# The lead-in of a fused attention and experts kernel in another order: loads on two queues, spans from index fills, one trigonometric stay, and products between TensorE's sums

## Chip, cores and metric

The kernel runs on one core of a Trainium2 chip. The metric is the device time of one execution in microseconds; lower is better.

## What is computed

Attention with a complex decay over 4 x 8 heads, 768 positions, 48 columns, in float32:

```
mag = sqrt(a_re*a_re + a_im*a_im);  scale = min(mag, 0.999) / (mag + 1e-6)
for t in range(S):                       # a = (a_re + i a_im) * scale
    S_re, S_im = a * (S_re + i S_im) + k[t] outer v[t]   # the product is real, added to S_re
    y[t] = q[t] @ S_re
```

Its output becomes 3072 rows of 384. Every row is given to one of 8 experts of 384 rows each, in the order of the scores `x @ w_gate`, and passes `relu(x @ w1[e]) @ w2[e]`. Last, all rows pass `((x @ w_a) * (x @ w_b)) @ w_out`.

## The kernel before, in words

The program has two blocks, attention and experts. The change is in the first (function `attention`, from L185), and there almost wholly in what each engine does ahead of its loop.

**Tiles.** A tile `g` is 128 positions of all 8 heads of one batch: 24 tiles. The recurrence inside of a tile is written as products. Decays are kept as logarithms: `log_r` (L1226) is the log of the clipped magnitude, its sums over positions are products with triangular constants (`to_mid`, `mid_to_end`, `spans`; L864, L868, L876), and `exp` of these sums scales queries and keys. The phase is summed in the same way in turns (`sum_phase`, L880 to L892: a product with `tri_turns`, one with `tri_half`, one with `last_row`), reduced to half a turn (L1246, L1250), and its sine and cosine turn queries and keys (L531, L532). Keys and queries are transposed (`turn`, L856), copied (L625, L626), scaled by the spans (`scale`, L1149 and three times L1162), and multiplied block by block at four distances (`gram_near`, L915, `gram8`, `gram16`, `gram32`, L926, L937, L947). `mask` (L1193) keeps the causal half.

**Pairs.** What depends on `a` alone is made for a pair `m` of tiles, 768 columns wide: squares (L680, L686), their sum (L1199), log (L652), magnitude (L663), log of the magnitude plus a small number (L657), the denominator |re| + magnitude (L667, L1205), its inverse as exp(-ln) with one correction (L672, L674, L1210, L1212), the ratio (L1256), its arctangent (L711), and the angle (L1240), with `left` (L1232) for the negative half plane.

**Order.** There is no scheduler. Each engine has a list written out by hand: `start()`, then a loop of ten passes with two tiles each (`body` with a late, a middle and an early tile), then `finish()`. Engines hand over by semaphores counted per tile or pair; an engine works through its own list in order, so a wait holds all that stands behind it. ScalarE's table holds either log and exp or sine and arctangent; `to_trig` and `to_exp` (L730, L733) load the other. The first body of TensorE begins with the turn of tile 1; that of VectorE with the scaling of tile 1.

**The lead-in.** SP issues the loads: pair 0 of `a` (four parts of 192 KB), pair 1, then `wg` and `w_out`'s first tile, and after a wait for VectorE's zeroing (`zeroed`) q, k and v of tiles 0 and 1. TensorE waits for `wg` ahead of its first product (L845). GpSimd makes all constants first: `first_constants`, `sum_constants`, `other_constants` (L258 to L279). The last of these makes `spans`, 66 columns of ones cut by 16 selects, each waiting for the one before. TensorE's first span sums wait for all of them (L1011, `const_made` at 3).

ScalarE's `start()` (L735) squares both halves of pairs 0 and 1, and makes pair 1's log and magnitude ahead of tile 0's decays; VectorE's is at L1259, TensorE's at L1007, GpSimd's at L575. The lines in question are these, with their surroundings:

## Time and profile before

| what | us |
|---|---|
| median of 3 runs | 1132.54 |
| the three runs | 1132.19, 1132.54, 1135.49 |
| the profiled execution, its own time | 1136.5 |
| its span, first to last instruction | 1134.8 |
| busy TensorE, VectorE, ScalarE, GpSimd | 1063.5, 813.2, 505.9, 446.9 |
| attention's loop, from and to about | 51, 383 |

A profile shows one execution. The page sums it up by engine, by slices of the span, by the chain that ended last and by groups of instructions. The order of time lists instructions with start, duration, line and tiles, and in brackets how long the engine had been idle and what ended that. The table of stretches gives each engine's busy time in stretches of the span, and the granted clock of TensorE, 1.00 for 2.4 GHz and 0.50 for 1.2 GHz.

### The profile page before, as it was taken

The numbers are of one execution on the slowest core, as the hardware profiler recorded it, in microseconds if no ns is written. First come the engines' busy times: TensorE is split into PE (matmuls) and PEld (weight loads), VectorE is DVE, ScalarE is ACT, GpSimd is POOL, SyncE is SP. The second block draws the span as 40 slices with busy tenths as digits, with TensorE's granted clock in tenths as the row PEclk, the third lists the DMA queues.
The fourth block names the chain that finished last, engine by engine and source line by source line (L and its number), as shares of the span: only waits on it lengthen the run. The fifth ranks groups of instructions, "written<-read, shape, count | busy, mean of one in ns | idle before, by whom it ended". The sixth has DMA issues, their size and how long they took to land.

```text
span 1134.8 us, 36403 instructions
## 1 busy us (share of the span) xinstructions
PE 1063.5 (94%) x14126; PEld 978.1 (86%) x14126; DVE 813.2 (72%) x1808; ACT 505.9 (45%) x951; POOL 446.9 (39%) x473
## 2 busy tenths in 40 slices
PE   1899999999999927899999999999999999999997
PEld 1578888888888816899999999999999999999997
DVE  5779999999998887865865865865864864874221
ACT  6767777777776332224323323323323323313322
POOL 7556565555566326703403403403403502502501
PEclk9989999999999958999999999999999999999999
DMA  6233444444433153030030030030030030030000
GB/s 133 57 69 83 88 90 90 90 90 90 90 85 83 32 174 133 29 115 19 21 111 22 21 111 22 21 111 22 21 111 22 21 111 22 14 118 22 21 1 21
DMA packets 163640, 73.99 MB, mean 65 GB/s; under 512 B 140016, under 2 KB 158192, under 8 KB 163568
## 3 DMA queue, kind: packets, MB, share of 16 engines
q1 hardware_dynamic: 160496, 63.73, 21.4%
q0 software_dynamic: 3072, 9.44, 2.6%
q8 instruction: 28, 0.46, 0.2%
q14 instruction: 44, 0.36, 0.1%
HBM read 63.71 MB, written 9.44 MB: 64 GB/s over the span
## 4 chain that ended last, share of the span: by engine, by line
PE 58%; DVE 3%; issue 1%; DMA 1%; ACT 0%; POOL 0%; SPq 0%; DVEq 0%; ACTq 0%; POOLq 0%
PE tb L2196 26%; PE acc L1837 7%; PE acc L1839 7%; PE acc L1838 7%; PE tb L1837 2%; PE tb L1839 2%; PE tb L1838 2%; PE ps_r L1747 1%; DVE slot L152 1%; DVE thr L145 1%; DMA w1s<-in_moe_w 1%; PE tb L1820 0%; PE tb L2149 0%; PE tb L2153 0%; PE tb L2150 0%
## 5 line engine op out<-in xcount | busy, mean ns | idle before, releaser
L2018 ACT CAST ab_high<-ab 128x384 fp32r<-128x384 f32 x96 | 49.4, 514 | 224.5 <-DVE ab L2103 211.0
L2103 DVE TENSOR_TENSOR ab<-tb,a_sb 128x384 f32<-128x384 f32 x96 | 53.3, 556 | 100.4 <-PE tb L2196 95.1
L1886 POOL TENSOR_TENSOR w_low<-w1s,w_high 128x384 fp32r<-128x384 f32 x64 | 65.6, 1034 | 144.2 <-ACT w_high L1963 144.2
L1810 POOL DMA_INDIRECT xg<-x_rows,tok_next x24 | 25.7, 1070 | 221.8 <-issue 221.5
L2196 PE MATMUL tb<-x_high,wb_high 128*128 128x384 f32 x288 | 99.7, 346 | 0.0
L1837 PE MATMUL acc<-wo_high,ab_high 128*128 128x384 f32 x288 | 98.2, 341 | 0.3 <-DVE ab_low L2106 0.3
L2196 PE MATMUL tb<-x_high,wa_high 128*128 128x384 f32 x288 | 97.5, 338 | 0.0
L1839 PE MATMUL acc<-wo_high,ab_low 128*128 128x384 f32 x288 | 97.4, 338 | 0.0
L1838 PE MATMUL acc<-wo_low,ab_high 128*128 128x384 f32 x288 | 97.1, 337 | 0.0
L2106 DVE TENSOR_TENSOR ab_low<-ab,ab_high 128x384 fp32r<-128x384 f32 x96 | 53.6, 558 | 60.1 <-ACT ab_high L2018 60.1
L2196 PE MATMUL tb<-x_high,wb_low 128*128 128x384 f32 x288 | 96.6, 335 | 0.0
L2196 PE MATMUL tb<-x_high,wa_low 128*128 128x384 f32 x288 | 96.5, 335 | 0.0
L2014 ACT COPY a_sb<-tb 128x384 f32<-128x384 f32 x96 | 46.0, 479 | 112.8 <-PE tb L2196 112.8
L1162 DVE TENSOR_TENSOR x<-ps_t,span_dec 112x512 f32<-112x512 f32 x144 | 90.0, 679 | 0.0
L152 DVE TENSOR_TENSOR slot<-best,thr 128x768 bf16<-128x768 f32 (+1 forms) x80 | 88.2, 1121 | 0.9
L557 POOL TENSOR_TENSOR kxt<-rot,to_end 128x384 f32<-128x384 f32 x48 | 48.4, 1032 | 100.5 <-DVE log_r L1226 50.3
L1892 POOL TENSOR_TENSOR w_low<-w2s,w_high 128x384 fp32r<-128x384 f32 x64 | 72.5, 1133 | 37.7 <-ACT w_high L1974 37.4
L2034 DVE SCALAR_TENSOR_TENSOR hid_low<-tb,hid_high 128x384 fp32r<-128x384 f32 x64 | 35.4, 554 | 58.3 <-ACT hid_high L2000 57.5
L1837 PE MATMUL acc<-hid_high,w_high 128*128 128x384 f32 x192 | 66.9, 349 | 1.4 <-DVE hid_low L2034 1.4
L524 POOL TENSOR_TENSOR qk_dec<-qk,dec 128x384 f32<-128x384 f32 x48 | 57.4, 1196 | 23.3 <-ACT dec L632 22.9
L2196 PE MATMUL tb<-x_low,wa_high 128*128 128x384 f32 x288 | 65.6, 335 | 0.0
L2196 PE MATMUL tb<-x_low,wb_high 128*128 128x384 f32 x288 | 65.4, 334 | 0.0
(371 smaller groups left out, 3019.0 us busy)
## 6 DMA issues: line engine op xcount, KB each, us to landing
w1s<-in_moe_w SPq DMA_DIRECT2D x8, 1536.0 KB, 6.4
w2s<-in_moe_w SPq DMA_DIRECT2D x8, 1152.0 KB, 9.4
a_re_in<-in_a_re SPq DMA_DIRECT2D x30, 192.0 KB, 3.1
a_im_in<-in_a_im SPq DMA_DIRECT2D x30, 192.0 KB, 3.7
qk<-in_q SPq DMA_DIRECT2D x24, 192.0 KB, 2.7
qk<-in_k SPq DMA_DIRECT2D x24, 192.0 KB, 3.3
vv<-in_v SPq DMA_DIRECT2D x48, 96.0 KB, 2.9
x_rows<-ysb SPq DMA_DIRECT2D x24, 192.0 KB, 3.0
```

The costliest lines, as they stand in the source:

```text
L152: return v.tensor_tensor(t["slot"][:, cols, :], scores[:, cols].unsqueeze(2).broadcast_to([P, n, NTH]), t["thr"][:, min(i, 1), :].unsqueez ...
L524: nc.gpsimd.tensor_tensor(qk_dec[:, :, cs], qk[:, u, :, cs], dec[:, :, cs], ALU.mult).then_inc(s["qk_decayed"], 1)
L1162: nc.vector.tensor_tensor(view(xw[n][:, hs, :]), mixed, by, ALU.mult).then_inc(s[f"scaled{w}"], 1)
L1837: nc.tensor.matmul(out_ap, left[0], right[0], start=start, stop=False)
L1838: nc.tensor.matmul(out_ap, left[0], right[1], start=False, stop=False)
L1839: return nc.tensor.matmul(out_ap, left[1], right[0], start=False, stop=stop)
L1886: nc.gpsimd.tensor_tensor(w1p[1][:, f % NW1, :, :], w1_tile(f), w1p[0][:, f % NW1, :, :].bitcast(F32), ALU.subtract).then_inc(s["w1_low"], 1)
L1892: nc.gpsimd.tensor_tensor(w2p[1][:, f % 2, :], w2s[:, f, :], w2p[0][:, f % 2, :].bitcast(F32), ALU.subtract).then_inc(s["w2_low"], 1)
L2018: nc.scalar.copy(abp[0][:, f % 2, :], ab[:, f % 2, :]).then_inc(s["ab_high"], 1)
L2103: nc.vector.tensor_tensor(ab[:, f % 2, :], tb[(2 * f + 1) % 4][:, 0:CAP], a_sb[:, f % 2, :], ALU.mult).then_inc(s["ab_made"], 1)
L2106: nc.vector.tensor_tensor(abp[1][:, f % 2, :], ab[:, f % 2, :], abp[0][:, f % 2, :].bitcast(F32), ALU.subtract).then_inc(s["ab_low"], 1)
L2196: mm = nc.tensor.matmul(tb[(2 * f + m) % 4][:, 0:CAP], w[:, k, :], x[:, k, :], start=(n == 0), stop=(n == len(terms) - 1))
```

## The change

- **Loads.** SP issues only the real parts of pair 0, then q and k of tile 0, then pair 1; ScalarE's queue issues the imaginary parts of pair 0 as its first act. q and k of tile 1 and the v loads come after `w_out`'s tile. The zeroing of `vv` is split in two halves and moved behind the first square sum and the second imaginary square on VectorE; each v load waits for its half.
- **Spans.** The 16 selects go. 16 index fills write two sides into a buffer that isn't in use yet, without waits between them; VectorE takes the minimum and compares with 0. TensorE waits for that (`spans_ready`) in place of all constants.
- **Squares.** VectorE makes the imaginary squares of pairs 0 and 1, ScalarE the rest.
- **ScalarE's list.** Inversion of pair 0 is split around the square of pair 1. Tile 0's decays and span decays come ahead of pair 1's size, log and magnitude. The two arctangents stand side by side; `log_magnitude_eps(1)` goes behind the reload of the log table; the size of pair 2 goes out of the stay with the sine table.
- **TensorE.** Six products of 384 columns whose result nobody reads, between the span sums and the first phase sum, and one between the two phase sums; some steps of tile 0 change places.
- **VectorE.** Another order of `start()`: the square sum of pair 2 behind the second angle, `log_twice_capped(2, 0)` ahead of `scale(0, 0, 1)`, `log_decay(1, 1)` ahead of `denominator(2)`, `left_side(2, 0)` and `square_sum(3)` last.
- **GpSimd.** Its wait for the ratio of pair 2 ahead of tile 1's keys goes.

The core of the diff:

```diff
@@ SP
-                load_a(sp, 0, 0, 0, 0)
+                load_part(sp, a_re, re_in, 0, 0, 0)
+                load_qk(sp, 0, 0, 0)
                 load_a(sp, 1, 0, 2, 1)
                 sp.dma_start(wg[:], w_gate.rearrange("(n p) e -> p n e", p=P)).then_inc(gate_loaded, 16)
                 load_wo(sp, 0)
-                sp.wait_ge(zeroed, 1)
+                load_qk(sp, 0, 1, 1)
                 for u in range(2):
-                    load_qk(sp, 0, u, u)
+                    sp.wait_ge(zeroed, u + 2)
                     load_v(sp, 0, u, u)
@@ GpSimd
                 def start():
                     sum_constants(pool)
+                    span_sides(pool, sides)
                     other_constants(pool)
...
                     queries_and_keys(1, 1, 0)
-                    pool.wait_ge(s["ratio_made"], after("ratio_made", 2))
                     keys_to_end(1, 1)
+    def span_sides(pool, sides):
+        def side(view, pattern, base, cm):
+            nc.gpsimd.iota(view, pattern=pattern, base=base, channel_multiplier=cm, **kw).then_inc(sides_made, 1)
@@ ScalarE
+                load_part(act, a_im, im_in, 0, 0, 0)
                 nc.scalar.preload_act_table_set("natural_log_exp_and_others")
...
                     square_re(0, 0)
-                    square_im(0, 0)
                     absolute(0, 0)
                     log_magnitude(0)
                     magnitude(0)
                     log_magnitude_eps(0)
+                    act.wait_ge(s["den_made"], after("den_made", 0))
+                    nc.scalar.activation(den_inv[:], den[:], ACT.Ln).then_inc(s["den_logged"], 1)
                     square_re(1, 1)
-                    square_im(1, 1)
-                    inverse(0)
+                    act.wait_ge(s["den_logged"], after("den_logged", 0))
+                    nc.scalar.activation(den_inv[:], den_inv[:], ACT.Exp, scale=-1.0).then_inc(s["log_den_inv"], 1)
+                    decays(0, 0)
+                    span_decays(0, 0, 0)
+                    span_decays(0, 0, 1)
+                    absolute(1, 1)
                     log_magnitude(1)
                     magnitude(1)
-                    decays(0, 0)
-                    log_magnitude_eps(1)
-                    absolute(1, 1)
-                    span_decays(0, 0, 0)
-                    span_decays(0, 0, 1)
                     inverse(1)
                     to_trig()
                     arctan(0)
+                    arctan(1)
                     square_re(2, 0)
+                    half_sines(0, first_sines)
                     square_im(2, 0)
-                    absolute(2, 0)
-                    arctan(1)
-                    half_sines(0, first_sines)
                     half_sines(1, s["sines_made"])
                     act.sem_inc(s["cos_abs"], 1)
                     copy_turned(0, 0)
                     to_exp()
-                    decays(1, 1)
+                    log_magnitude_eps(1)
+                    decay_to_mid(1)
                     copy_turned(0, 1)
+                    decay_of_end(1)
+                    absolute(2, 0)
                     span_decays(1, 1, 0)
                     log_magnitude(2)
+                    span_decays(1, 1, 1)
                     magnitude(2)
-                    span_decays(1, 1, 1)
@@ TensorE
+                def keep_running(products):
+                    for _ in range(products):
+                        nc.tensor.matmul(ps_u[:, 0, 0:HD], to_mid[:], log_r[:, 0, :], start=True, stop=True)
...
-                    pe.wait_ge(const_made, 3)
+                    pe.wait_ge(spans_ready, 2)
                     sum_spans(0, 0, 0)
                     pe.wait_ge(s["ends_made"], after("ends_made", 0))
                     sum_spans(0, 0, 1)
+                    keep_running(FIRST_RUN)
                     sum_phase(0, 0, None, ps_y)
+                    keep_running(1)
                     sum_phase(0, 1, None, ps_y)
                     sum_mids(1, 1, 0)
                     sum_ends(1, 1)
                     turn(0, 0)
+                    gram_near(0, 0)
                     sum_phase(1, 0, None, ps_y)
-                    gram_near(0, 0)
+                    turn(0, 1)
                     gram8(0, 0)
                     gram16(0, 0)
-                    turn(0, 1)
                     gram32(0, 0)
@@ VectorE
+                def make_spans():
+                    dve.wait_ge(sides_made, 4 * len(LEVELS) + 4)
+                    nc.vector.tensor_tensor(spans[:], sides[0], sides[1], ALU.min).then_inc(spans_ready, 1)
+                    dve.wait_ge(spans_ready, 1)
+                    nc.vector.tensor_scalar(spans[:], spans[:], 0.0, None, ALU.is_ge).then_inc(spans_ready, 1)
                 def start():
+                    square_im(0, 0)
                     square_sum(0)
+                    nc.vector.memset(vv[:, 0, :, :, :], 0.0).then_inc(zeroed, 1)
+                    log_twice_capped(0, 0)
                     denominator(0)
-                    log_twice_capped(0, 0)
                     log_decay(0, 0)
+                    left_side(0, 0)
+                    square_im(1, 1)
+                    nc.vector.memset(vv[:, 1, :, :, :], 0.0).then_inc(zeroed, 1)
+                    make_spans()
+                    invert(0)
                     square_sum(1)
-                    invert(0)
                     ratio(0, 0)
-                    left_side(0, 0)
+                    denominator(1)
                     log_twice_capped(1, 1)
-                    denominator(1)
                     invert(1)
                     angle(0)
                     ratio(1, 1)
-                    square_sum(2)
                     reduce_phase(0, 0, ps_y)
                     reduce_phase(0, 1, ps_y)
                     left_side(1, 1)
                     angle(1)
+                    square_sum(2)
                     scale(0, 0, 0)
                     reduce_phase(1, 0, ps_y)
+                    log_twice_capped(2, 0)
                     scale(0, 0, 1)
                     reduce_phase(1, 1, ps_y)
+                    log_decay(1, 1)
                     denominator(2)
-                    log_decay(1, 1)
-                    log_twice_capped(2, 0)
                     dve.wait_ge(const_made, 3)
                     mask(0)
-                    square_sum(3)
-                    left_side(2, 0)
                     invert(2)
                     ratio(2, 0)
+                    left_side(2, 0)
+                    square_sum(3)
```

`FIRST_RUN` is 6.

## Rows read from the trace of the kernel before

**Rows 1.** The page, part 4: the chain that ended last, shares by engine.

```profile
PE 58%; DVE 3%; issue 1%; DMA 1%; ACT 0%; POOL 0%; SPq 0%; DVEq 0%; ACTq 0%; POOLq 0%
```

**Rows 2.** Table of stretches: us, busy us per engine (instructions), granted clock, DMA share, GB/s.

```profile
75.00:103.50 28.50, 28.19 (x798) 23.15 (x797) 26.09 (x38) 21.62 (x38) 18.98 (x17) 1.00 0.40 88
```

**Rows 3.** Order of time, VectorE: start us, duration us, line, operation; log_r.

```profile
49.49 0.95 DVE L1226 SCALAR_TENSOR_TENSOR log_r<-log_twice,log_mag_eps 128x768 f32<-128x768 f32 x1
...
87.86 0.95 DVE L1226 SCALAR_TENSOR_TENSOR log_r<-log_twice,log_mag_eps 128x768 f32<-128x768 f32 x1
...
354.98 0.95 DVE L1226 SCALAR_TENSOR_TENSOR log_r<-log_twice,log_mag_eps 128x768 f32<-128x768 f32 x1
```

**Rows 4.** Table of stretches of 2 us in the first pass.

```profile
58.00:60.00 2.00, 1.74 (x49) 1.64 (x41) 1.88 (x4) 1.63 (x4) 0.84 (x2) 0.50 1.14 223
...
68.00:70.00 2.00, 1.99 (x94) 1.86 (x91) 1.88 (x4) 0.39 (x1) 0.00 (x0) 1.00 0.72 179
```

**Rows 5.** Order of time, TensorE, in the first and the second pass.

```profile
53.20 0.81 PE L868 MATMUL ps_r<-log_r,mid_to_end 128*128 128x384 f32 x2
...
54.69 0.69 PE L915 MATMUL ps_s<-qd,kd 112*64 112x64 f32 x16 [0.69 <-ACT kd L626]
...
57.37 0.74 PE L926 MATMUL ps_s<-x 112*8 112x8 f32 x64 [1.98 <-DVE x L1162]
...
58.64 1.95 PE L856 MATMUL ps_t<-ident,rot 128*112 128x128 f32 x8 [0.26 <-DVE x L1162]
...
66.44 1.18 PE L891 MATMUL ps_r<-phase,last_row 128*128 128x384 f32 x2
...
92.34 1.08 PE L856 MATMUL ps_t<-ident,rot 128*112 128x128 f32 x8
...
96.64 0.81 PE L891 MATMUL ps_r<-phase,last_row 128*128 128x384 f32 x2
```

**Rows 6.** The first load: order of time, and one row of the stretches.

```profile
2.09 1.95 SPq L432 DMA_DIRECT2D a_im_in<-in_a_im  x2
...
2.18 1.28 ACT L617 ACT_TABLE_LOAD   x1 [2.18 <-issue]
...
3.50:4.00 0.50, 0.00 (x0) 0.00 (x0) 0.47 (x3) 0.00 (x0) 0.43 (x2) 1.00 1.09 216
```

**Rows 7.** Order of time from the first square to the first span sums.

```profile
6.69 0.84 ACT L680 ACTIVATE mag<-a_re_in 128x768 f32<-128x768 f32 x1 [3.23 <-DMA a_im_in<-in_a_im]
...
8.93 9.71 POOL L222 TENSOR_SCALAR_AFFINE_SELECT spans<-spans 128x8 f32<-128x8 f32 x16
...
13.09 0.96 DVE L1226 SCALAR_TENSOR_TENSOR log_r<-log_twice,log_mag_eps 128x768 f32<-128x768 f32 x1
...
21.29 1.15 PE L876 MATMUL ps_e<-spans,log_r 128*64 128x66 f32 x16 [4.09 <-POOLq L279]
...
24.58 0.14 POOL L166 IOTA weight<- 128x8 f32 x1
```

**Rows 8.** Order of time, first angle, and one phase sum at either level.

```profile
25.37 1.28 ACT L730 ACT_TABLE_LOAD   x1
...
27.60 0.96 DVE L1240 SCALAR_TENSOR_TENSOR theta<-left,arc 128x768 f32<-128x768 bf16 x1 [0.26 <-ACT arc L711]
...
28.61 1.65 PE L889 MATMUL ps_y<-theta,tri_turns 128*128 128x384 f32 x2 [5.29 <-DVE theta L1240]
...
30.37 1.49 PE L891 MATMUL ps_y<-phase,last_row 128*128 128x384 f32 x2
...
45.73 0.91 PE L889 MATMUL ps_y<-theta,tri_turns 128*128 128x384 f32 x2
```

**Rows 9.** Order of time, tile 0 copied and scaled, tile 1 scaled.

```profile
38.98 0.56 ACT L625 COPY qd<-ps_t 112x512 f32<-112x512 f32 x1
...
44.69 0.69 DVE L1149 TENSOR_TENSOR qs<-ps_t,span_dec 112x512 f32<-112x512 f32 x1 [1.49 <-ACT qd L625]
...
56.03 0.68 DVE L1149 TENSOR_TENSOR qs<-ps_t,span_dec 112x512 f32<-112x512 f32 x1
```

More of the change, by code:

```diff
@@ L51 @@
 WARM_UP = 16
+FIRST_RUN = 6
 BETWEEN_TILES = (2, 2, 1)
@@ L299, in attention @@
         turns = sbi("turns", [P, HD])
+        sides = [turns[:, n * NSPAN:(n + 1) * NSPAN] for n in range(2)]
         cos_sin = sbi("cos_sin", [P, 2, 2, HD])
@@ L416, in load_v, with load_part @@
                     sp.dma_start(vv[ts, u, :, j, :], src[ts, :, :]).then_inc(v_loaded[u], 16)
+            def load_part(eng, x, dst, b, c, parity):
+                for i in range(2):
+                    to = dst[:, parity, i, :] if isinstance(parity, int) else \
+                        dst[:, bass.ds(parity, 1), i, :].rearrange("p o n -> p (o n)")
+                    eng.dma_start(to.rearrange("p (h d) -> p h d", h=H), chunk(x, b, c if i == 0 else c + 1)
+                                  ).then_inc(a_loaded, 16)
             def load_a(sp, m, b, c, parity):
@@ L428, in load_a @@
                 for x, dst in zip((a_re, a_im), a_in):
[L429 to L433 removed]
+                    load_part(sp, x, dst, b, c, parity)
             def store(sp, g, u):
```

47 lines of the change are left out of this document (26 added, 21 removed).

## The prediction, made before the changed kernel ran

> **What bounds the kernel now.** I read the page first, then the table of stretches, then the order of time of the lead-in. On the page the chain that ended last is 58% TensorE [rows 1]: the second half, the experts, is a TensorE stream that the change doesn't touch. The attention loop decides what a lead-in is worth. Its stretches are full on TensorE (28.19 of 28.50 us) with VectorE close behind (26.09) [rows 2], so each engine takes from the lead-in only a starting time, and one microsecond of later start is one microsecond of later end. The pace is in log_r, made once per pass: 49.49, 87.86, and nine passes later 354.98 [rows 3]. Later passes take (354.98 - 87.86) / 9 = 29.68 us, the first 38.37, so 8.7 us are lost in it. Where, is in the clock column: 0.50 at 58 to 60, 1.00 at 68 to 70 [rows 4]. Ahead of that fall TensorE has little to do: the sums of ends finish at 54.01, 0.69 us of products stand at 54.69, and the next begin at 57.37, 1.98 us of that wait for VectorE's scaled tile [rows 5]. The fall's price comes from the same work in two passes [rows 5]: from the turn at 58.64 to the end of the phase sums at 67.62 is 8.98 us, from 92.34 to 97.45 it is 5.11. So **the fall costs 3.9 us**. Note that the clock column shows 1.00 at 3.5 us as well [rows 6], ahead of TensorE's first product and of any record; a product of one shape takes 1.65 us at 28.61 and 0.91 at 45.73 [rows 8], so TensorE still stood at its lower level (1.2 GHz) at 28.61.
>
> **The change, step by step.** Times are from the start of the profiled span; "now" is the trace.
> 1. First load. Now SP issues all four parts, the last two from 2.09 on, and the first square starts at 6.69 [rows 6, 7]. At 3.5 to 4.0 us the DMA engines move 216 GB/s at a share of 1.09 [rows 6]: they are full, and 0.197 MB takes 0.9 us. Issuing from two queues can't speed up what the engines bound. ACT can't issue ahead of 2.18 [rows 6], and SP now sends q and k of tile 0 (0.39 MB) in between. Bounds: landing as now (6.65) if these stay behind, 8.5 if both go ahead (2 x 0.9 more). I take 8.0, as they alternate. The Trainium skill (DMA: Bandwidth & Descriptors, Queues, rings and completion order) says that each engine goes round the queues with work packet by packet; by that rule, as an estimate, the two loads on ACT's queue land near 7.8, and the sum would be 0.2 us better.
> 2. To the first log_r. Now the step from the square at 6.69 to log_r's end at 14.05 takes 7.36 [rows 7]. With the imaginary square on VectorE beside ScalarE's, and the capped log ahead of the denominator: three VectorE steps of 0.96 and three of ScalarE near 0.87, with their hand-overs 5.8 us: 13.8. TensorE can't start earlier, for wg is behind the second load on SP, which waits for the first: 1.35 later than now. TensorE starts at 14.2, as now to 0.1 us. Gain here: nothing. VectorE's two added squares (1.9 us) and the zeroing of vv (1.3 us, in two halves, moved from ahead of the load to behind it) lie in its waits for ScalarE; without these waits they would cost 3.2 us.
> 3. Spans. Now 16 selects hold GpSimd for 9.71 us and the span sums start at 21.29 [rows 7]. Sixteen index fills at 0.14 to 0.2 us each [rows 7] take 3.2 at most and are made by 12; the small minimum and compare on VectorE, not in the trace, are bounded by 0.1 and 0.5 each; I take 0.12, as the width is 66 against the 768 of a 0.96 us step. They are done by 16.2, hidden behind the decays, which end near 16.9. Span sums start at 16.9 and end by 19.0: **4.3 us earlier**.
> 4. But the second pair's size, log and magnitude are put behind these spans on ScalarE. Size 19.4, log 20.2, magnitude 21.1 to 21.9, denominator to 22.9, two inversions to 24.6, table load (1.28) to 25.9, arctangent, angle to 27.7; now it ends at 27.60 + 0.96 = 28.56 [rows 8]. **Of 4.3 us 0.85 are left.**
> 5. TensorE kept running: a phase sum is five passes of 384 columns and takes 3.25 us now, 28.61 to 31.86 [rows 8], so 0.65 a pass at the lower level. Six products of two passes take 7.8, from 19.0 to 26.8, ahead of the angle at 27.7: cover 0.9 us, and if it goes, what is over is a delay. Now TensorE is idle for 5.29 us ahead of 28.61 [rows 8] and both phase sums of tile 0's pair run at the lower level; with TensorE busy from 17 on I take the clock as full when the first one starts. Each then takes 0.91/1.65 of 3.25, 1.8 us: 2.9 us for two. Turning of tile 0's first half ends at 35.35, where it is 38.9 now (its copy starts at 38.98 [rows 9]): 3.5 us earlier.
> 6. What is late next: VectorE's second scaling of tile 0. Now it starts at 44.69 [rows 9]. The change puts log_twice of pair 2 ahead of it. On ScalarE stand, from 35.4: two copies, table load, the log moved out of the first stay, two decays (to 39.3), two copies to 40.8, the end decay, a size, a span decay, then pair 2's log, ending at 43.1. log_twice ends at 44.1, and the scaling starts there: **0.6 us ahead of now**; the other 2.9 us are VectorE's new wait.
> 7. The tail of the lead-in to the scaling of tile 1 is now 44.69 to 56.03, 11.3 us of full VectorE [rows 9]. After: 2.5 scaling, 1.1 reduction, log_r, denominator, mask to 50.0; then it waits for two ScalarE inversions (1.8 us behind a denominator that comes second instead of first) until 51.2, three steps to 54.1, side and square sum: 55.4. Again 0.6 ahead. The same walk made for the kernel before gives 55.1 where the trace has 56.0, so it is up to 0.9 short; if that lag is whole in the new order too, this is a loss of 0.3. I take the middle, **-0.2 us**, with -1.5 (first load as now) and +1.6 (latest load, whole lag) as ends.
> 8. At nothing: the wait that GpSimd loses (tile 1's keys are wanted only by the state's products late in the first pass), and the v loads, each now behind its half of the zeroing (the later at 15.7) and behind it the loads of pair 2: these wait for pair 0's ratio at 19.6 as well and land near 25.3, where the first square of pair 2 stands at 29.5. That is a cover of 4 us; if it goes, ScalarE waits with the sines behind it.
>
> Against the profiled execution's own 1136.5 the sum is 1136.3, the fall left in. The median of the runs shown is 4.0 us lower than that execution, and of three runs two lie at 1132.2 and 1132.5 and one at 1135.5. That is the size of the fall, so perhaps the fall isn't in each execution; the runs have no trace to show it. The median goes to 1132.54 - 0.2 = 1132.3.
>
> **Rivals.**
> Slower: the fall comes in nearly every execution. In the new order TensorE is through with the sums of ends by about 52, two microseconds sooner, since log_r is made ahead of the denominator; the next big work is still bound to VectorE's scaling at 55.4, so it begins near 56.8. The poor stretch is 4.8 us with 0.7 of products in it, where it is 3.4 now [rows 5]. If the runs at 1132 had no fall, it adds 3.9: 1136.2. It decides where that stretch is longer than now. For it: the arithmetic of steps 6 and 7. Against: two of three runs of before may have passed such a stretch without a fall. The Trainium skill (TensorE: Matmul & The Clock Gate, HAM oscillation) says that waits between bursts bring the lower level back, each time anew; by that rule too the time is that of this rival, and rows 4 and 5 agree with it at one place.
> Faster: the fall goes, because with the clock full early TensorE's work lies elsewhere, and the median of before had it (the profile's 4.0 us then being the profiler's). 1132.3 - 3.9 = 1128.4. For it: the fall stands behind one stretch only, and a scaling of tile 1 that comes two microseconds sooner than step 7 has it would close that stretch. Against: step 7 finds no such gain.
> The products don't do what they are for: the clock is still at the lower level in both phase sums. Then the 2.9 us of step 5 come back: 1135.2. Against: TensorE is busy from 17 on, where now it is idle until 28.6.
>
> **How the numbers follow.** Forecast 0.46 (own range 1130.8 to 1134.1), slower rival 0.27, faster rival 0.22, idle products 0.05. A measurement of this kernel tells 0.3% (3.4 us) from no change: under 1129.1 is faster, over 1135.9 slower. The slower rival lies on that line, 0.17 of it beyond; with the 0.05 slower is 0.22 at most. Faster is the rival and 0.03 of the forecast's tail: 0.25. The rest, 0.53, is the same. The range takes in both rivals' times: 1128.0 to 1136.8.
>
> **What would show it.** In the new profile: first square at 7.8 to 8.2 (step 1); span sums by 17.5 (3); first angle ending near 27.7 (4); phase sums under 1.8 us from the first on (5); VectorE idle some 3 us until log_twice near 43, second scaling at 44 (6); scaling of tile 1 at 55.4 to 56.4 (7); and the clock column between 50 and 70, with the first pass's 38.4 us, says which rival holds. Wrong would be a first pass that starts before 54 or after 57.5, or a later pass that isn't 29.7 us long: then the lead-in does something to the loop that I haven't seen.

## The result, and the profile after

| | before | after |
|---|---|---|
| median (8 executions each, in turn on one chip) | 1133.24 us | 1137.80 us |
| range | 1132.19 to 1135.49 | 1135.23 to 1140.25 |
| ratio after / before | | 1.0038, 95% interval 1.0024 to 1.0052 |
| profiled execution, own time / span | 1136.5 / 1134.8 | 1139.83 / 1138.1 |
| mean granted clock of that execution | 0.979 | 0.975 |

The change makes the kernel slower by 0.38%, some 4.3 us. I had forecast 1132.3, range 1128.0 to 1136.8; the result lies outside. Of the 5.5 us between forecast and result 0.7 are the base, since the kernel before took 1133.24 here. Measured once more on another chip (the run after_again below) the ratio is 1.0034 [1.0021, 1.0046].

The page of after, parts 1, 2 and 4. Every engine has nearly the work it had, and the chain's shares are those of [rows 1].

```profile
PE 1070.7 (94%) x14140; PEld 983.0 (86%) x14140; DVE 816.3 (72%) x1813; ACT 505.6 (44%) x949; POOL 442.2 (39%) x472
...
PEclk9889999999999967999999999999999999999999
...
PE 58%; DVE 3%; issue 2%; DMA 1%; POOL 0%; ACT 0%; DVEq 0%; POOLq 0%; ACTq 0%; SPq 0%
```

First load to first span sums, order of time. These rows answer to [rows 6, 7].

```profile
2.18 1.08 ACTq L431 DMA_DIRECT2D a_im_in<-in_a_im  x2
...
7.67 0.84 ACT L700 ACTIVATE mag<-a_re_in 128x768 f32<-128x768 f32 x1 [3.10 <-DMA a_im_in<-in_a_im]
...
9.29 1.94 POOL L265 IOTA turns<- 128x8 f32 x16 [0.17 <-POOL end_bias L258]
...
12.49 0.96 DVE L1253 SCALAR_TENSOR_TENSOR log_r<-log_twice,log_mag_eps 128x768 f32<-128x768 f32 x1
...
13.71 1.62 PE L886 MATMUL ps_e<-log_r,to_mid 128*128 128x384 f32 x2 [13.71 <-POOLq L287]
15.56 0.16 DVE L1294 TENSOR_TENSOR spans<-turns 128x66 f32<-128x66 f32 x1
15.76 0.20 DVE L1296 TENSOR_SCALAR spans<-spans 128x66 f32<-128x66 f32 x1
...
16.54 1.15 PE L898 MATMUL ps_e<-spans,log_r 128*64 128x66 f32 x16
```

Pair 1's steps, the products and the first phase sum; they answer to [rows 8]. The two VectorE steps of 1.64 and 1.75 us take 0.95 elsewhere; GpSimd's `qk_dec` runs beside them.

```profile
16.41 2.94 POOL L537 TENSOR_TENSOR qk_dec<-qk,dec 128x384 f32<-128x384 f32 x2 [2.85 <-ACT dec L650]
...
16.85 1.64 DVE L1239 SCALAR_TENSOR_TENSOR den_inv<-den,den_inv 128x768 f32<-128x768 f32 x1
...
18.41 1.75 DVE L1226 SCALAR_TENSOR_TENSOR mag<-mag,im 128x768 f32<-128x768 f32 x1
18.50 4.75 PE L1031 MATMUL ps_u<-log_r,to_mid 128*128 128x384 f32 x12
...
26.98 0.96 DVE L1267 SCALAR_TENSOR_TENSOR theta<-left,arc 128x768 f32<-128x768 bf16 x1 [0.26 <-ACT arc L731]
...
27.99 1.65 PE L911 MATMUL ps_y<-theta,tri_turns 128*128 128x384 f32 x2 [4.75 <-DVE theta L1267]
```

Now the place where the time goes. It answers to [rows 9] and [rows 3].

```profile
36.48 1.65 DVE L1267 SCALAR_TENSOR_TENSOR theta<-left,arc 128x768 f32<-128x768 bf16 x1
...
37.27 1.72 POOL L545 TENSOR_TENSOR rot<-qk_dec,cos_sin 128x384 f32<-128x384 f32 x1
38.05 1.76 DVE L1226 SCALAR_TENSOR_TENSOR mag<-mag,im 128x768 f32<-128x768 f32 x1
38.94 2.69 POOL L570 TENSOR_TENSOR kxt<-rot,to_end 128x384 f32<-128x384 f32 x2
39.73 0.68 DVE L1176 TENSOR_TENSOR qs<-ps_t,span_dec 112x512 f32<-112x512 f32 x1
...
42.25 1.09 PE L878 MATMUL ps_t<-ident,rot 128*112 128x128 f32 x8 [1.52 <-DVE x L1189]
...
43.38 0.59 ACT L639 COPY qd<-ps_t 112x512 f32<-112x512 f32 x1 [2.03 <-PE ps_t L878]
...
45.82 0.86 ACT L672 ACTIVATE log_mag<-mag 128x768 f32<-128x768 f32 x1
...
46.71 1.06 DVE L1245 SCALAR_TENSOR_TENSOR log_twice<-log_mag 128x768 f32<-128x768 f32 x1 [3.46 <-ACT log_mag L672]
47.69 0.68 DVE L1176 TENSOR_TENSOR qs<-ps_t,span_dec 112x512 f32<-112x512 f32 x1
...
51.14 0.95 DVE L1253 SCALAR_TENSOR_TENSOR log_r<-log_twice,log_mag_eps 128x768 f32<-128x768 f32 x1
...
58.94 0.68 DVE L1176 TENSOR_TENSOR qs<-ps_t,span_dec 112x512 f32<-112x512 f32 x1
...
89.44 0.95 DVE L1253 SCALAR_TENSOR_TENSOR log_r<-log_twice,log_mag_eps 128x768 f32<-128x768 f32 x1
...
356.55 0.95 DVE L1253 SCALAR_TENSOR_TENSOR log_r<-log_twice,log_mag_eps 128x768 f32<-128x768 f32 x1
```

Read it backwards. The second scaling of tile 0 starts at 47.69, where it was 44.69. It stands behind `log_twice`, which waits 3.46 us for ScalarE's log of pair 2. That log is late because ScalarE's two copies before it wait for TensorE's second turn. The turn waits for VectorE's first scaling, and that one stands behind an angle and a square sum of 1.65 and 1.76 us, beside GpSimd's `rot` and `kxt`. In the kernel before, the same copies and the same log stood at nearly the same time:

```profile
44.07 0.58 ACT L625 COPY qd<-ps_t 112x512 f32<-112x512 f32 x1 [1.40 <-PE ps_t L856]
...
45.65 0.83 ACT L652 ACTIVATE log_mag<-mag 128x768 f32<-128x768 f32 x1
```

There the scaling waited for the copies alone. What is new is that it waits for the log as well.

From the second scaling on the lag stays: tile 1 is scaled at 58.94 (56.03 before). At `log_r`, which now stands ahead of the denominator, the lag is smaller: 1.65 us at the first of the loop (51.14 against 49.49) and still 1.57 at the last (356.55 against 354.98). So the loop itself has its old pace, (356.55 - 89.44) / 9 = 29.68 us a pass.

The span has grown by 3.3 us, though, so 1.7 us more are lost **behind** the last `log_r`, in work the change doesn't touch. The tables of stretches, after and then before, show what is different there: the clock falls once more, where it didn't before.

```profile
394.00:396.00 2.00, 1.34 (x10) 1.37 (x11) 1.86 (x4) 0.00 (x0) 0.00 (x0) 0.81 0.02 6
396.00:398.00 2.00, 2.00 (x20) 1.83 (x21) 0.47 (x1) 0.00 (x0) 0.00 (x0) 0.50 0.03 8
```

```profile
392.00:394.00 2.00, 2.00 (x35) 1.91 (x34) 1.36 (x3) 0.00 (x0) 0.00 (x0) 1.00 0.00 0
```

It falls in the state's products, which wait 1.13 us for VectorE in both kernels: 16 of them take 2.76 us in after and 1.78 before.

```profile
394.66 2.76 PE L922 MATMUL ps_u<-vv,kxt 128*112 128x96 f32 x16 [1.13 <-DVE state L1211]
```

```profile
391.72 1.78 PE L900 MATMUL ps_u<-vv,kxt 128*112 128x96 f32 x16 [1.13 <-DVE state L1184]
```

### The profile page after: what moved, and what is told of

It reads as the page before. It is cut to its first block, busy times and chain, and to the rows that moved or that the text cites. A ratio compares the mean times of both kernels' runs of the same rounds, so it can differ in the third digit from the quotient of the medians.

```text
span 1138.1 us, 36431 instructions
## 1 busy us (share of the span) xinstructions
PE 1070.7 (94%) x14140; PEld 983.0 (86%) x14140; DVE 816.3 (72%) x1813; ACT 505.6 (44%) x949; POOL 442.2 (39%) x472
## 4 chain that ended last, share of the span: by engine, by line
PE 58%; DVE 3%; issue 2%; DMA 1%; POOL 0%; ACT 0%; DVEq 0%; POOLq 0%; ACTq 0%; SPq 0%
PE tb L2240 27%; PE acc L1881 7%; PE acc L1883 7%; PE acc L1882 7%; PE tb L1881 2%; PE tb L1883 2%; PE tb L1882 2%; PE ps_r L1791 1%; DVE slot L153 1%; DVE thr L146 0%; PE tb L1864 0%; PE tb L2193 0%; PE tb L2197 0%; PE tb L2194 0%; DMA w2s<-in_moe_w 0%
## 5 line engine op out<-in xcount | busy, mean ns | idle before, releaser
L2078 DVE SCALAR_TENSOR_TENSOR hid_low<-tb,hid_high 128x384 fp32r<-128x384 f32 x64 | 35.5, 555 | 58.4 <-ACT hid_high L2044 57.5
```

## The experiments

Four theories. **Order**: VectorE's two moves (the square sum of pair 2 ahead of the first scaling, `log_twice` ahead of the second) cost it. **Port**: VectorE's steps with two inputs in SBUF meet GpSimd. **Clock**: TensorE's poor stretches bring the lower level back, ahead of the loop and near 395. **Products**: the six products are too few, or harmful. Each kernel was timed in five rounds beside the kernel before on the same chip. An execution of the kernel before took 1129.7 to 1140.9 us in these jobs, with medians from 1134.2 to 1135.1, so ratios within 0.002 of each other aren't told apart. Ratio and median can differ by up to 0.0013, as in undo_three; the argument goes by the ratio. The last three columns come from one profiled execution each.

| run | ratio [95%] | median | 2nd scaling of tile 0 | tile 1 scaled | last log_r |
|---|---|---|---|---|---|
| (before, profiled execution) | 1 | | 44.69 | 56.03 | 354.98 |
| (after, first measurement) | 1.0038 [1.0024, 1.0052] | 1137.80 | 47.69 | 58.94 | 356.55 |
| after_again | 1.0034 [1.0021, 1.0046] | 1138.81 | 48.05 | 59.29 | 356.88 |
| twice_back | 1.0028 [1.0016, 1.0041] | 1137.35 | 44.23 | 57.50 | 357.00 |
| square_back | 1.0046 [1.0030, 1.0062] | 1140.45 | 47.28 | 58.78 | 358.17 |
| undo_two | 1.0015 [0.9996, 1.0034] | 1137.07 | 44.14 | 57.20 | 353.65 |
| undo_three | 1.0003 [0.9985, 1.0021] | 1136.64 | 43.43 | 57.16 | 355.97 |
| undo_four | 1.0010 [0.9992, 1.0028] | 1135.02 | 42.86 | 56.18 | 352.08 |
| wait_alone | 1.0013 [0.9995, 1.0030] | 1136.23 | 48.28 | 58.27 | 358.25 |
| no_products | 1.0051 [1.0031, 1.0071] | 1141.21 | 49.04 | 60.28 | 357.05 |
| twelve_products | 1.0031 [1.0016, 1.0045] | 1137.88 | 47.00 | 58.26 | 357.06 |
| after_fill | 1.0039 [1.0025, 1.0054] | 1139.19 | 47.78 | 59.03 | 354.66 |
| undo_four_fill | 1.0014 [1.0000, 1.0028] | 1137.04 | 43.87 | 55.77 | 352.06 |
| loads_alone | 0.9995 [0.9978, 1.0012] | 1134.62 | 44.93 | 56.28 | 355.49 |
| scalar_order_alone | 0.9988 [0.9976, 1.0001] | 1134.55 | 43.09 | 55.76 | 352.51 |
| spans_alone | 0.9980 [0.9963, 0.9996] | 1132.96 | 43.24 | 54.58 | 353.90 |
| spans_fill | 0.9980 [0.9963, 0.9997] | 1132.52 | 44.84 | 56.19 | 351.96 |
| spans_products | 0.9993 [0.9976, 1.0010] | 1133.64 | 41.18 | 52.61 | 351.55 |
| fill_alone | 0.9988 [0.9973, 1.0004] | 1131.84 | 41.93 | 53.36 | 349.43 |
| spans_early_fill | 0.9986 [0.9971, 1.0001] | 1132.02 | 41.81 | 53.25 | 349.10 |

### VectorE's order, taken back step by step

**twice_back** takes the first move back in the changed kernel:

```diff
                     reduce_phase(1, 0, ps_y)
-                    log_twice_capped(2, 0)
                     scale(0, 0, 1)
...
                     denominator(2)
+                    log_twice_capped(2, 0)
```

> The changed kernel with one thing undone: log_twice of pair 2 stands behind denominator(2) on VectorE again. Order theory: the second scaling of tile 0 (47.69 in the changed kernel's profile, 44.69 before) waits for nothing but the copies and starts near 44.5, the first scaling of tile 1 near 56, and the median falls by about 3 us against the changed kernel, to 1134.5 to 1135.5. Clock theory (the loss lies in more falls of TensorE's clock, the order costs nothing): the second scaling moves, the time stays above 1137.

The second scaling comes back to 44.23, so the wait was that move. Of 3.5 us only 1.4 are left at tile 1: `log_twice` now takes its 1 us there, and VectorE met GpSimd, so that its denominator took 1.76 us instead of 0.95. The last `log_r` isn't earlier at all (357.00): the first pass takes 41.2 us in this profile, with TensorE's lower level from 56 to 70.

```profile
48.00 2.69 POOL L570 TENSOR_TENSOR kxt<-rot,to_end 128x384 f32<-128x384 f32 x2
...
49.76 1.76 DVE L1232 TENSOR_TENSOR den<-den,mag 128x768 f32<-128x768 f32 x1
```

**square_back** takes the other move back alone:

```diff
                     angle(1)
-                    square_sum(2)
                     scale(0, 0, 0)
+                    square_sum(2)
```

> The changed kernel with square_sum(2) put behind scale(0, 0, 0) on VectorE. In the changed kernel it takes 1.76 us in front of that scaling, which holds the second turn of tile 0 on TensorE. Order theory: first scaling at 38.1 in place of 39.73, second turn, its copies, and so the log of pair 2 and the second scaling 1.6 us sooner (46.1): 1.6 us off the median, to 1136. Clock theory: the same instructions sooner, the time within 0.7 us of the changed kernel's.

The first scaling is 1.5 us earlier (38.24), the second 0.4: the wait for the log still rules.

```profile
41.89 0.59 ACT L639 COPY qd<-ps_t 112x512 f32<-112x512 f32 x1 [0.36 <-PE ps_t L878]
...
45.05 0.83 ACT L672 ACTIVATE log_mag<-mag 128x768 f32<-128x768 f32 x1
```

The copies come 1.5 us sooner and the log only 0.8, since a span decay ahead of it waits for TensorE's sums of tile 1; `log_twice` itself took 1.45 us. So the slow square sum holds the copies, but it is the smaller part of the wait. Nothing is won; its ratio is the second worst of all.

**undo_two** is twice_back and GpSimd's wait:

```diff
                     queries_and_keys(1, 1, 0)
+                    pool.wait_ge(s["ratio_made"], after("ratio_made", 2))
                     keys_to_end(1, 1)
```

> The changed kernel with two things undone: log_twice of pair 2 behind denominator(2), and GpSimd again waits for the ratio of pair 2 ahead of tile 1's keys. In the run with the first alone, denominator(2) took 1.76 us in place of 0.95 and log_r 1.17, while GpSimd made these keys. Order theory: both are back at 0.95, the first scaling of tile 1 starts at 56.2 (57.5 with the first alone, 58.94 in the changed kernel), and the median is 1 us under that run's 1137.35. Clock theory: no change of the median, 1137 to 1138.

The denominator is back at 0.95, but GpSimd's step moved 7 us later and there met the square sum of pair 3:

```profile
55.33 2.80 POOL L570 TENSOR_TENSOR kxt<-rot,to_end 128x384 f32<-128x384 f32 x2 [7.23 <-DVE arc L1284]
55.51 1.77 DVE L1227 SCALAR_TENSOR_TENSOR mag<-mag,im 128x768 f32<-128x768 f32 x1
```

**undo_three** also puts `square_sum(2)` back behind the first scaling. **undo_four** also has the last steps of VectorE's list in their old order, out of the way of GpSimd's step:

```diff
+                    square_sum(3)
+                    left_side(2, 0)
                     invert(2)
                     ratio(2, 0)
-                    left_side(2, 0)
-                    square_sum(3)
```

> As the run before it, with square_sum(2) behind scale(0, 0, 0) as well. Order theory: the second turn of tile 0 comes 1.5 us sooner (40.7), the second scaling at 42.7, the first scaling of tile 1 near 55.0, a microsecond ahead of the kernel before; the median is that of before or 1 us less, 1133 to 1134.5. Clock theory: above 1136.5.

> The run that undid three things, and a fourth undone: square_sum(3) and left_side(2, 0) ahead of the inversion of pair 2 again. In that run the square sum took 1.77 us beside GpSimd's keys of tile 1, which the ratio of pair 2 had just let go, and VectorE's first scaling of tile 1 started at 57.16 although the second of tile 0 was at 43.43. Order theory (VectorE's steps with two SBUF inputs are 0.8 us longer when GpSimd works beside them, and the new order puts them there): the square sum is back at 0.95 and lies ahead, the first scaling of tile 1 starts at 55.0, the median is 1.5 us under before's or more. Clock theory: same median as that run within 0.5 us (1.0003 of before).

Together the steps bring the ratio from 1.0034 to 1.0038 down to 1.0003 to 1.0010, some 3 to 4 us. In the trace tile 1 comes back to 56.18, not to 55.0: the denominator met GpSimd once more and took 1.76 us. No single step of this ladder is outside the noise; from the changed kernel to undo_four it is, and so is the cleanest pair, on one chip in one job: after_fill at 1.0039 [1.0025, 1.0054] against undo_four_fill at 1.0014 [1.0000, 1.0028].

**wait_alone** goes the other way: the two moves of VectorE, and nothing else, in the kernel before.

```diff
-                    square_sum(2)
...
                     angle(1)
+                    square_sum(2)
                     scale(0, 0, 0)
                     reduce_phase(1, 0, ps_y)
+                    log_twice_capped(2, 0)
                     scale(0, 0, 1)
...
-                    log_twice_capped(2, 0)
```

> The kernel before with two of the change's moves on VectorE alone: log_twice_capped(2, 0) ahead of the second scaling of tile 0, and square_sum(2) behind the second angle. ScalarE's log of pair 2 ends at 46.5 us in the kernel before. If this wait is the main cause: second scaling at 47.3 to 47.6 in place of 44.69, scaling of tile 1 at 57.5 to 59 in place of 56.03, ratio 1.0015 to 1.003. If the wait is covered (TensorE has enough else to do): ratio within 0.001 of 1.

The trace repeats the picture of the changed kernel, row by row:

```profile
46.94 1.42 DVE L1218 SCALAR_TENSOR_TENSOR log_twice<-log_mag 128x768 f32<-128x768 f32 x1 [2.28 <-ACT log_mag L652]
48.28 0.68 DVE L1149 TENSOR_TENSOR qs<-ps_t,span_dec 112x512 f32<-112x512 f32 x1
```

The second scaling is 3.6 us later than before, tile 1's 2.2, the last `log_r` 3.3. The median rises by 1.2 us, with an interval that just reaches no change. So the moves are shown to cost their microseconds in the lead-in. At the median they may be some 30% of the loss; the interval allows nothing as well as most of it.

### The products

**no_products** and **twelve_products**, both in the changed kernel:

```diff
-FIRST_RUN = 6
+FIRST_RUN = 0
...
-                    keep_running(1)
```

```diff
-FIRST_RUN = 6
+FIRST_RUN = 12
```

> The changed kernel without the six products and the one between the phase sums. Order theory: in the profile TensorE's clock had fallen again before the first phase sum, so the products gave only the second one 1 us; without them the second scaling is at most 1 us later and the median 0 to 1 us higher. Clock theory: the early rise and fall are what shifts the later falls; without the products the time is that of before within 1 us, 1133 to 1134.

> The changed kernel with 12 products in place of 6: they reach to about 27.6, up to the angle at 27.98, so that the clock stays at its full level. Order theory: both phase sums at 1.8 us or less in place of 3.3 and 2.1; the turn of tile 0 some 2 us sooner and the second scaling with it (45.7): 1135.5 to 1136. If the clock then falls elsewhere for it (clock theory), the gain is gone again: 1137 or more.

With none, both phase sums of the first pair run at the lower level and all is 1.3 us later in the trace: the products do pay there. The ratio, 1.0051, isn't told apart from the changed kernel's. With twelve, TensorE is busy until 26.75 and the first phase sum has the full clock, but the level fell at 38 instead, and again at 59:

```profile
28.80 0.91 PE L911 MATMUL ps_y<-theta,tri_turns 128*128 128x384 f32 x2 [2.06 <-DVE theta L1267]
```

```profile
38.00:40.00 2.00, 2.00 (x17) 1.14 (x13) 2.00 (x3) 1.99 (x3) 2.00 (x3) 0.61 0.93 182
```

VectorE's second scaling still stands behind the log, at 47.00, only 0.7 us earlier, and the time is that of the changed kernel.

### The parts alone, in the kernel before

**loads_alone** has the loads of the change, with the zeroing left whole and where it was:

```diff
-                load_a(sp, 0, 0, 0, 0)
+                load_part(sp, a_re, re_in, 0, 0, 0)
+                load_qk(sp, 0, 0, 0)
...
+                load_qk(sp, 0, 1, 1)
                 sp.wait_ge(zeroed, 1)
...
+                load_part(act, a_im, im_in, 0, 0, 0)
```

> The kernel before with the load part alone: imaginary parts of pair 0 from ScalarE's queue, q and k of tile 0 in between, q and k of tile 1 ahead of the v loads. Both theories: the first square starts 1.0 us later than before (7.67 in the changed kernel against 6.69), and since ScalarE still makes both squares the first log_r and all behind it too: 1 us slower than before at most, 0 if the wait for GpSimd's constants at 21.29 takes it up, which I expect: within 0.5 us of before.

**spans_alone** has index fills, minimum and compare for the 16 selects:

```diff
                     sum_constants(pool)
+                    span_sides(pool, sides)
...
-                    pe.wait_ge(const_made, 3)
+                    pe.wait_ge(spans_ready, 2)
...
                     log_decay(0, 0)
+                    make_spans()
```

> The kernel before with the index fills alone. Order theory: the span sums start at 18.4, behind the decays, in place of 21.29; ScalarE's 2.5 us wait for them goes, and the first angle starts 2.3 us sooner (25.3); TensorE is at its lower level until the phase sums, as before; the second scaling is 2 us sooner and the time 2 us under before's. Clock theory: an earlier start shifts the falls, and the median is not under before's by more than 0.5 us.

**scalar_order_alone** has ScalarE's new list from the first arctangent to `magnitude(2)`, as in the diff of the change, and on VectorE `square_sum(2)` behind the first scaling:

```diff
-                    log_magnitude_eps(1)
...
                     arctan(0)
+                    arctan(1)
                     square_re(2, 0)
+                    half_sines(0, first_sines)
                     square_im(2, 0)
-                    absolute(2, 0)
-                    arctan(1)
-                    half_sines(0, first_sines)
...
```

> The kernel before with ScalarE's new order from the first arctangent on (both arctangents side by side, log_magnitude_eps(1) behind the reload, the size of pair 2 out of the stay), and square_sum(2) behind the first scaling, since it can't stand ahead of the reductions any more. If ScalarE's order is what is left of the loss: tile 1's scaling 0.5 to 1.5 us later and ratio 1.001 to 1.002. If it is neutral, as I held in the prediction: both angles 0 to 1 us earlier, tile 1's scaling within 0.7 us, ratio 0.999 to 1.001.

The loads are neutral: the first square starts at 7.87 instead of 6.69, the first scaling of tile 1 0.25 us later. The spans are the good part of the change, the one edit whose interval lies below 1:

```profile
17.67 1.15 PE L885 MATMUL ps_e<-spans,log_r 128*64 128x66 f32 x16 [0.70 <-ACT dec L641]
...
26.14 0.96 DVE L1249 SCALAR_TENSOR_TENSOR theta<-left,arc 128x768 f32<-128x768 bf16 x1 [0.26 <-ACT arc L720]
...
54.58 0.68 DVE L1158 TENSOR_TENSOR qs<-ps_t,span_dec 112x512 f32<-112x512 f32 x1
```

The sums come 3.6 us earlier (21.29 before), the angle 1.46 (27.60), tile 1 1.45 (56.03), the median 1.9. ScalarE's order from the first arctangent on is neutral or better, so it isn't what is left of the loss. Its earlier part (tile 0's decays ahead of pair 1's log, the split inversion) was not tried alone.

### The clock

**fill_alone** puts three products at the end of TensorE's list ahead of the loop, in the kernel before; **spans_fill** adds the index fills, **spans_products** has the index fills, ten products ahead of the first phase sum and one between the two, **spans_early_fill** all three. **after_fill** and **undo_four_fill** have the three products on top of the changed kernel and of undo_four.

```diff
                     pe.wait_ge(s["reduced"], after("reduced", 1, 2))
+                    for _ in range(3):
+                        nc.tensor.matmul(ps_y[:, 0:HD], to_mid[:], tri_turns[:].unsqueeze(1).broadcast_to([P, 3, P]),
+                                         start=True, stop=True)
```

> The kernel before with the index fills, 10 products behind the span sums and one between the phase sums. In the run with the fills alone (0.9980 of before) the phase sums were at the lower level. Order theory: they fall to 1.8 us each, the first scaling of tile 1 comes 2 to 3 us sooner than with the fills alone (52.5), 0.996 of before. If VectorE is what bounds the lead-in behind the first angle, it comes at 54 and nothing is gained over the fills alone. Clock theory: the clock falls once more in the first 50 us and the gain is lost.

> The kernel before with the index fills and three products (into a free bank, 384 columns of a constant) at the end of TensorE's start list, ahead of the turn of tile 1. They move the turn by 2.2 us, inside its slack, and leave less than 1 us of the poor stretch. The fall of the clock in the first pass goes: granted clock 1.00 from 36 to 390 us, the first pass is 34 to 35 us long in place of 38.3, and the time is 3 to 4 us under that with the fills alone, 0.9945 of before. If the fall isn't in most executions without a profile, the gain is smaller, about 1.5 us.

> The kernel before with the same three products alone. The fall's price measured by itself: in the trace the first pass shrinks from 38.4 to 34.5 us, in the median 2 to 4 us, 0.9970 of before. The forecast's slower rival lives on this price; if the median doesn't move, the fall cannot explain any of the changed kernel's loss.

> The changed kernel once more, unedited, beside the three below. Theory (the loss is order and clock falls, both part of the kernel): ratio 1.003 to 1.005 as before, some 4 us. Rival (the first measurement met a bad chip or a bad stretch of time): under 1.002. It is the base for what the edits below give.

> The changed kernel with three products of 384 columns at the end of TensorE's list ahead of the loop, nothing else. If some 1.5 to 2.5 us of the loss is the clock falling in TensorE's poor stretch ahead of the loop and again around 395: ratio 1.001 to 1.0025, and no fall in the trace between 40 and 390. If the loss is the order on VectorE and GpSimd alone: within 0.001 of the unedited kernel of the same job.

> The changed kernel with all four steps of order on VectorE and GpSimd put back, and the three products. If order and clock falls are the whole loss and add up: ratio 0.997 to 0.9995, since the index fills' gain of 0.002 is then left. If something else of the change costs (ScalarE's order, TensorE's order, the loads): above 1.000.

> The kernel before with the index fills, ten products between span sums and first phase sum, one between the phase sums, and three at the end of TensorE's list ahead of the loop: every stretch of TensorE that was poor ahead of the loop is filled. If the clock falls are what kept the earlier start (tile 1 scaled at 52.6 instead of 56.0) from reaching the end: ratio 0.995 to 0.997, 1128.5 to 1131. If the earlier start is lost elsewhere: 0.998 to 1.000, like the fills alone.

The filling does to the trace what it is for. The table of stretches of spans_fill, where the kernel before has 0.85 and 0.64:

```profile
50.00:60.00 10.00, 8.41 (x165) 6.33 (x165) 9.81 (x15) 9.04 (x14) 2.35 (x3) 1.00 0.26 51
60.00:70.00 10.00, 9.40 (x265) 7.85 (x260) 8.53 (x12) 5.83 (x10) 6.47 (x6) 1.00 0.48 100
```

The first pass, from `log_r` to `log_r`, falls from 38.4 to 35.2 us. But the medians hardly follow: spans_fill has the ratio of spans_alone, after_fill that of after_again, and fill_alone's 0.9988 reaches 1. (Its profiled execution flatters it: GpSimd's 16 selects took 8.08 us there and 9.71 in [rows 7], and its first angle is 1.6 us earlier for that reason. So most of its 2.7 us at tile 1 isn't the products' doing, which run at 47.73.) spans_early_fill is 2.8 us below the kernel before at the median, but its ratio is 0.9986, within noise of spans_alone. **Faster than both kernels** are spans_alone and spans_fill, by 0.2% against before and some 0.55% against after.

Where do an earlier loop's microseconds go? I took the span less the start of the last `log_r` from each profile, and counted the falls of the clock that stand between 385 and 500 beside the long one, of 34 to 38 us from 395 to 406 on, which all have.

| further falls | profiles | span - last log_r, us |
|---|---|---|
| none | before, spans_alone, spans_fill, fill_alone, spans_early_fill, loads_alone, scalar_order_alone, square_back, undo_three, undo_four | 777.8 to 781.4, mean 779.8 |
| one (388 to 395, or 479 to 483) | after, after_again, after_fill, twice_back, twelve_products, spans_products, wait_alone | 779.6 to 782.8, mean 781.1 |
| two (both places) | no_products, undo_two, undo_four_fill | 783.6 to 784.7, mean 784.0 |

By these means one further fall goes with 1.3 us and two with 4.2, but the ranges of none and one overlap, and something else differs too. Near 480 TensorE waits for VectorE's `slot`: 1.9 to 2.0 us in 13 of the profiles, 0.2 to 0.4 in the other 7. Among the profiles without a further fall the long wait goes with 1.6 us more (780.4 against 778.8). Between profiles with equal waits, one fall goes with 1.1 to 1.5 us and two with 3.6. The first fall comes behind a wait of 1.0 to 1.1 us that 19 of the 20 have, and 8 of them fell. The one near 480 comes only behind the long wait, in 5 of those 13. Order of time, in after_again, then in before, then in after:

```profile
479.85 0.47 PE L1791 MATMUL ps_r<-choice,slot 128*128 128x16 bf16 x12 [2.01 <-DVE slot L153]
```

```profile
477.00 0.47 PE L1747 MATMUL ps_r<-choice,slot 128*128 128x16 bf16 x12 [1.90 <-DVE slot L152]
```

```profile
480.05 0.47 PE L1791 MATMUL ps_r<-choice,slot 128*128 128x16 bf16 x12 [0.16 <-DVE slot L153]
```

A stretch 2 to 5 us behind it, in the first two of these: the lower level in the one, the full one in the other.

```profile
482.00:484.00 2.00, 2.00 (x8) 2.00 (x7) 1.67 (x8) 0.00 (x0) 0.00 (x0) 0.50 0.00 0
```

```profile
480.00:482.00 2.00, 2.00 (x14) 2.00 (x13) 1.30 (x5) 0.41 (x1) 0.00 (x0) 1.00 0.00 0
```

Of the 11 profiles with the changed start, 8 have such a fall; of the 9 of the kernel before and those built on it, 2. That difference points the right way: undo_four_fill has its last `log_r` 2.9 us ahead of before and ends 2.0 us behind it. It isn't shown to be the whole: square_back has no such fall, and its ratio is 1.0046. **Why** the changed kernels meet these falls more often isn't settled. One execution per kernel is too few. TensorE's own new order, the imaginary squares on VectorE and the early part of ScalarE's list were not tried alone either, and with the index fills worth 0.0020 and the four steps undone at 1.0010, some 0.003 of ratio, 3.4 us, stays with them or with the falls.

## Why the prediction was wrong, point by point

1. **Load.** First square 7.67 (I held 7.8 to 8.2), behind a landing at 7.57 (I took 8.0). The Trainium skill's rule (DMA: Bandwidth & Descriptors, Queues, rings and completion order) gave 7.8 as an estimate for that landing, and the trace is near it. The size is right, and the loads are neutral by loads_alone.
2. **First log_r.** It ends at 13.45 (held 13.8), TensorE starts at 13.71 (14.2). `wg` had landed at 13.40, but TensorE starts 0.26 us behind the end of `log_r`, as before (0.25 behind 14.05). The constants' signal that the profile names there, L287, is the third, and TensorE's list waits for the second. Right in size, wrong in cause.
3. **Spans.** 16 fills take 1.94 us, minimum and compare 0.16 and 0.20, the sums start at 16.54 (16.9). Right.
4. **Pair 1.** The first angle ends at 27.94 (27.7), 0.6 us ahead of before. Right. spans_alone shows what the rest of the change gives away: with ScalarE's old order the same index fills have it at 27.10.
5. **Products.** Wrong. I had priced each of them at the lower level and 19.0 to 26.8 busy. They took 4.75 us, 18.50 to 23.25, as the clock rose on the way; then TensorE was idle for 4.75 us, the level fell, and the first phase sum took 1.65 us again. A filler that speeds itself up ends early. Of the 3.5 us that I held for tile 0's first half 1.7 came (its copy at 37.27 against 38.98): the angle was 0.6 us earlier, and the level rose again within the second phase sum.
6. **The step that failed**, the path to pair 2's log: "two copies to 40.8 ... pair 2's log, ending at 43.1. log_twice ends at 44.1." The copies ran from 43.38 to 44.45, the log ended at 46.68, the second scaling started at 47.69: 3.6 us later than held. I had walked ScalarE's list alone, and left out that the second turn on TensorE can't start before VectorE has scaled the first half (42.25, released by that scaling). In the trace of before that log ends at 46.48. The walk held it 3.4 us earlier; it came 0.2 later, and `log_twice` now makes the scaling wait for it. The first scaling in turn stands behind two VectorE steps for which the walk had no term. They took 1.65 and 1.76 beside GpSimd's `rot` and `kxt`. They aren't the larger part: with the square sum moved away (square_back) the log still ended at 45.88, 2.8 us later than held. The 1.65 stands in the trace of before too, at the second angle (38.10); [rows 3, 7, 8] show such a step at 0.95 to 0.96, and that was my only price. The Trainium skill (SBUF — State Buffer, SBUF: two separate sides) says that a VectorE operation with two inputs in SBUF and a GpSimd operation that reads SBUF share a pair of ports by an exclusive lock, so that one waits for the whole of the other. The rows agree: 0.95 becomes 1.64 to 1.77 where such a step meets GpSimd's `qk_dec`, `rot` or `kxt` for long, and GpSimd's own steps go from 1.01 to 1.33 and 1.72.
7. **To tile 1.** 47.69 to 58.94 is 11.25 us; I had 44.1 to 55.4, 11.3. Right; the whole miss of 3.5 us at tile 1 comes from step 6. It is also past the 57.5 that I named as wrong.
8. **At nothing.** In the changed kernel GpSimd's lost wait costs nothing in the trace: `kxt` is through at 50.56, and the denominator at 52.00 takes 0.95. It isn't free in twice_back, where it lets `kxt` run beside the denominator, and its restored wait puts `kxt` beside another step (undo_two). The difference of these two, 0.0013 in the ratio, is within noise. ScalarE's square of pair 2 didn't wait for its load.

**The fall.** I took the scatter of three runs for executions with and without the fall ahead of the loop. The recorded clock can tell. In each execution 2 x (1 - mean clock) x span is the recorded time at the lower level. Over the kernel before it is 48 to 53 us in the mean of a job, and 39 to 42 where the three products took that fall away from it (fill_alone, spans_fill, spans_early_fill). The changed kernel has 54 in after_again, and still 49 in after_fill. Most executions of before have the fall, but not all: 33 of the 145 in the five jobs have at most 41 us, which the long fall and a stretch at the kernel's end (34.1 and 4.7 us in the profile of before) use up. These 33 end 2.0 us below their job's median on average, so the scatter is in part what I took it for. The slower rival's 1136.2 lies near the result by luck. Its cause is out: after_fill removes the fall and stays at 1.0039. Its price of 3.9 us is near what the first pass pays in the trace (3.2 us by spans_fill); in the kernels with the three products it doesn't reach the end of the kernel at that size, for a reason that stays open.

The sum of the profiled execution: +3.0 at the second scaling (held -0.6), +2.9 at tile 1, +1.6 at the last `log_r`, +1.7 behind it, 3.3 in all (held -0.2).

## What to carry to other kernels

Before a step is moved ahead of another in a list written by hand, walk back from what it waits for, through every engine, to the point where the list meets itself: here VectorE waited for a log that waited for a turn that waited for VectorE. Price a step that will run beside GpSimd by a row in which it does so, not by the row where it is alone. And try a change's parts one by one: one part of this one, the index fills, was worth 1.9 us, and what was packed around it cost more than twice that.

## What was not expected of the hardware

- Products that keep TensorE busy are paid at the lower level for a while only: six products of two passes took 4.75 us, twelve 8.01, so what twelve took above six was 3.26, 0.27 us a pass where I had priced 0.65.
- The early fillers moved a fall rather than ended it: with six it stood at 27 to 33 us, with twelve at 38 to 42, with ten in the old order not before 53. With ten and the three ahead of the loop (spans_early_fill) TensorE kept the full level from 24 to 396 us, and the ratio was 0.9986.
- An idle stretch of 1.9 to 2.0 us on TensorE near 480 was followed by the lower level in 5 of 13 profiles.
- GpSimd's 16 chained selects took 9.71 us in one execution and 8.08 in another of the same code; 16 index fills without waits between them took 1.94.
